# Gates made in two groups, a 128-row recurrence, rest rows in two matmuls, and another order of VectorE's work beside an expert

## The chip, the cores and the metric

The kernel runs on one core of a Trainium2 chip (trn2). The metric is the device time of one execution in microseconds. The engines are TensorE (PE; PEld is its weight load), VectorE (DVE), ScalarE (ACT), GpSimd (POOL) and SyncE (SP), which here only issues DMAs.

## What is computed

An mLSTM recurrence, then a mixture of experts with a capacity, then a dense layer pair with a leaky activation:

```python
# q, k, v, o_gate: (4, 8, 768, 40); i_gate, f_gate: (4, 8, 768)
for t in range(S):
    m_new = max(f[t] + m, i[t]);  fs = exp(f[t] + m - m_new);  ist = exp(i[t] - m_new);  m = m_new
    C = fs * C + ist * outer(v[t], k[t]);  n = fs * n + ist * k[t]
    y[t] = sigmoid(o[t]) * (C @ q[t]) / max(|n . q[t]|, 1)
# x = y as (3072, 320); logits = x @ w_gate (320, 8)
# tokens go to experts greedily by falling logit, 384 tokens an expert
# out[mask] = relu(x[mask] @ w1[e]) @ w2[e]          (320 -> 1024 -> 320)
# then h = x @ w_in; (max(h,0) + alpha*min(h,0)) @ w_out   (320 -> 2048 -> 320)
```

## The kernel before

The sequence is cut into 6 chunks of 128 positions; with 4 batches there are 24 tiles (T = 4c + b) of 128 tokens and 8 heads. The program is written engine by engine, each with its own instruction order, and held together by semaphores. A `Chain` makes an engine wait for its own earlier result.

**Gates.** VectorE scans the gates of all 32 (batch, head) rows over 768 positions (lines 984 to 1012), ScalarE takes two Exps (845, 846), TensorE turns the results (568) and VectorE copies them. GpSimd clears the tiles' buffers and makes constants (420 to 469) before its first product. The decay exponents need the peak in three bf16 parts (`peak3`), one matmul against a selecting column each (588).

**Recurrence.** `over_chunks` runs a step for each tile: chunk 0 written out, chunks 1 to 4 in a loop, chunk 5 written out. In a step TensorE makes the decay exponents and scores of the next tile (`front`, 588 and 595), then for this tile the product with the carried state (617), the state's update (623), the router of two tiles ago (606) and the products with v (633), and turns the previous tile's row (642). ScalarE makes the decays (861), copies turned rows and sends them (868 to 872), and casts a sixteenth of `w_in` and `w_out` to the high part (899 to 903); its queue issues these raw weights, four loads a chunk (`load_raw`). VectorE makes probs (1039), the sum and the state (1059 to 1068) and the row x (1073 to 1079). GpSimd weighs v (478), masks (484), fades the state (490) and makes low parts (498 to 506). SyncE loads a tile with nine DMAs (383 to 387) once it has been used up. Head pairs lie in partitions 0 to 39 and 64 to 103. The o gates come in six large loads on ScalarE's queue and get a Sigmoid each before the rest.

**Routing.** VectorE turns the logits into two integer keys (1100 to 1120). In ten rounds compare (1138, 1140) -> count (667) -> blocks (1146) -> sum (673) -> flag (1155) -> base (679) the limit is found at which an expert is full; then its tokens are listed (1178 to 1217), their rows fetched by indirect DMA (532) and its weights loaded (406 to 410). The rounds of the next expert run between the matmuls of the one that is computed.

**Expert.** Every product of two fp32 matrices is made of fp32r parts, high times high, low times high and high times low: `parts3` (726 to 728) is three matmuls. The feature size 320 is two blocks of 128 and a rest of 64. On the way up the rest block holds high part and low part in its two halves, so it takes two matmuls (742, 743). The first layer's output product `down1` has three output tiles of 128 columns, the third being the rest twice, and each takes `parts3`. An expert has 8 steps of the first layer (`up`, `down1`) and 16 of the second (`up`, `down2`). ScalarE takes Relu and casts to the high part, VectorE makes the low part (`split_hidden`, 1266, 1271, 1276). At the end of an expert VectorE also makes the next keys (`reopen`, `best`), the low parts of the next expert's weights (`low_in` 1246 and 1248, `low_out` 1254) and rows (`rows_lo` 1258). TensorE turns the next expert's rows in three parts through one bank (`turn_rows`, 720), the next part only once `rows_lo` of the one before is done; then comes `first_up`.

```python
if more and 9 <= j < 12:
    low_in(e + 1, j - 9)
if more and 12 <= j < 15:
    rows_lo(e + 1, j - 12)
if more and 12 <= j < 15:
    low_out(e + 1, j - 12)
```

## Time and profile before

| | us |
|---|---|
| three runs | 891.87, 900.04, 902.94 (median 900.04) |
| the profiled execution | 891.99 |
| its span, first to last instruction | 890.1 |
| TensorE busy | 782.2 (88%) |
| VectorE busy | 597.9 (67%) |
| ScalarE busy | 318.0 (36%) |
| GpSimd busy | 166.9 (19%) |
| recurrence, to the last logits | 0 to 196.6 |
| first routing and first fetch | 196.6 to 248.6 |
| each of the six middle experts | 80.2 to 80.3 |

Durations come from the one profiled execution. Matmuls overlap, so the time from one start to the next is what counts, not the duration of one. The idle time that a row shows in square brackets lies before it, and the name behind the arrow is what ended it.

### The profile page before, as it was taken

How to read it: one execution, taken by the hardware profiler on the slowest of the kernel's cores; microseconds unless marked ns; L12 is line 12 of the kernel's file. 1: busy time of each engine (PE TensorE's matmuls, PEld its weight loads, DVE VectorE, ACT ScalarE, POOL GpSimd, SP SyncE). 2: the span in 40 equal slices, each digit the busy share in tenths (PEclk: the TensorE clock that was granted, in tenths of full speed). 3: DMA queues.
4: the chain of work that ended last, by engine and by line, in shares of the span. 5: the costliest groups of instructions: out<-in, count | busy, mean ns of one | idle time of the engine just before them, and what ended most of it. 6: DMA issues, size and time to landing. Idle time of an engine off the chain costs nothing.

```text
span 890.1 us, 16834 instructions
## 1 busy us (share of the span) xinstructions
PE 782.2 (88%) x5518; PEld 725.4 (82%) x5518; DVE 597.9 (67%) x1465; ACT 318.0 (36%) x732; POOL 166.9 (19%) x241
## 2 busy tenths in 40 slices
PE   1979999972199989998998999899989989998995
PEld 1878899961088978897897889889978988897995
DVE  7647678856766785777677677767766786775342
ACT  5426555510122441343235134313522441343331
POOL 8427667600100011011001101100110011011001
PEclk9989999975589999999999999999999999999998
DMA  9788887510500400050041005002300400050000
GB/s 250 157 203 193 205 195 173 136 36 1 168 1 1 143 28 23 7 163 22 0 133 35 22 0 159 24 7 67 101 22 0 141 27 22 1 167 23 1 1 22
DMA packets 102510, 68.52 MB, mean 77 GB/s; under 512 B 67984, under 2 KB 92048, under 8 KB 102480
## 3 DMA queue, kind: packets, MB, share of 16 engines
q1 hardware_dynamic: 85872, 45.05, 20.0%
q10 hardware_dynamic: 13920, 14.42, 5.5%
q0 software_dynamic: 2688, 8.65, 3.1%
q8 instruction: 17, 0.28, 0.1%
q14 instruction: 13, 0.11, 0.0%
HBM read 59.46 MB, written 8.65 MB: 77 GB/s over the span
## 4 chain that ended last, share of the span: by engine, by line
PE 51%; DVE 20%; issue 11%; ACT 8%; SPq 4%; DMA 3%; ACTq 1%; POOL 1%; DVEq 0%; POOLq 0%
PE bank L726 12%; PE bank L728 9%; PE bank L727 9%; DVE g_act L1271 6%; ACT h_hi L952 4%; PE bank L595 4%; PE bank L633 4%; PE bank L742 3%; PE bank L743 2%; DMA s<-w 2%; DVE w_lo L1254 2%; PE bank L667 2%; PE bank L617 2%; DVE by_row L1208 1%; PE bank L606 1%
## 5 line engine op out<-in xcount | busy, mean ns | idle before, releaser
L952 ACT CAST h_hi<-g_act 128x384 fp32r<-128x384 f32 x128 | 65.7, 514 | 188.3 <-DVE g_act L1271 188.3
L726 PE MATMUL bank<-wo_hi,h_hi 128*128 128x320 f32 x384 | 122.8, 320 | 0.6 <-DVE h_lo L1276 0.6
L728 PE MATMUL bank<-wo_hi,h_lo 128*128 128x320 f32 x384 | 120.1, 313 | 0.0
L727 PE MATMUL bank<-wo_lo,h_hi 128*128 128x320 f32 x384 | 119.5, 311 | 0.0
L532 POOL DMA_INDIRECT xe<-x_rows,idx_in x24 | 27.9, 1161 | 451.7 <-DVE idx_in L1216 393.3
L1276 DVE TENSOR_TENSOR h_lo<-g_act,h_hi 128x384 fp32r<-128x384 f32 x128 | 71.5, 559 | 59.8 <-ACT h_hi L952 58.0
L1271 DVE SCALAR_TENSOR_TENSOR g_act<-g_neg,rest_alpha,bank 128x384 f32<-128x384 f32 x128 | 78.3, 612 | 21.8 <-ACT g_neg L950 20.6
L726 PE MATMUL bank<-yT_hi,wi_hi 128*128 128x384 f32 x256 | 92.1, 360 | 0.1
L948 ACT ACTIVATE h_hi<-bank 128x384 fp32r<-128x384 f32 x64 | 31.5, 492 | 169.4 <-PE bank L743 169.4
L728 PE MATMUL bank<-yT_hi,wi_lo 128*128 128x384 f32 x256 | 86.6, 338 | 0.0
L727 PE MATMUL bank<-yT_lo,wi_hi 128*128 128x384 f32 x256 | 86.6, 338 | 0.0
L726 PEld LDWEIGHTS bank<-wo_hi,h_hi 128*128 128x128 f32 x384 | 73.4, 191 | 1.0 <-DVE h_lo L1276 0.9
L727 PEld LDWEIGHTS bank<-wo_lo,h_hi 128*128 128x128 f32 x384 | 73.4, 191 | 0.0
L728 PEld LDWEIGHTS bank<-wo_hi,h_lo 128*128 128x128 f32 x384 | 73.3, 191 | 0.0
L950 ACT ACTIVATE g_neg<-bank 128x384 f32<-128x384 f32 x128 | 62.6, 489 | 29.4 <-PE bank L743 28.7
L726 PE MATMUL bank<-h_hi,w_hi 128*128 128x384 f32 x192 | 69.9, 364 | 0.0
L728 PE MATMUL bank<-h_hi,w_lo 128*128 128x384 f32 x192 | 64.7, 337 | 0.0
L727 PE MATMUL bank<-h_lo,w_hi 128*128 128x384 f32 x192 | 64.4, 335 | 0.0
L543 POOL DMA_INDIRECT out<-out_sb,idx_out x24 | 27.3, 1138 | 190.0 <-DVE out_sb L1334 185.1
L861 ACT ACTIVATE decay<-bank,aT 128x128 f32<-128x128 f32 x192 | 51.5, 367 | 13.8 <-PE bank L588 9.6
L595 PE MATMUL bank<-q_wide,k_in 128*128 128x256 f32 x192 | 52.0, 418 | 1.6 <-DVE probs L1039 1.6
L726 PE MATMUL bank<-xT_hi,w_hi 128*128 128x384 f32 x128 | 51.6, 403 | 1.2 <-DVE xT_lo L1258 1.2
(208 smaller groups left out, 1776.8 us busy)
## 6 DMA issues: line engine op xcount, KB each, us to landing
s<-w SPq DMA_DIRECT2D x8, 1280.0 KB, 9.3
s<-w SPq DMA_DIRECT2D x8, 1024.0 KB, 5.4
s<-w SPq DMA_DIRECT2D x24, 256.0 KB, 6.5
sig<-o ACTq DMA_DIRECT2D x6, 640.0 KB, 8.5
q_in<-qT SPq DMA_DIRECT2D x48, 80.0 KB
q_wide<-qT SPq DMA_DIRECT2D x48, 80.0 KB
k_in<-kT SPq DMA_DIRECT2D x48, 80.0 KB
k_row<-k SPq DMA_DIRECT2D x48, 80.0 KB
```

What stands on the lines that cost most here:

```text
L532: pool.indirect_dma_start(xe[:, t, :], None, x_rows[:, :], bass.IndirectOffsetOnAxis(ap=idx_in[:, t:t + 1], axis=0)).then_inc(rows_in, 16)
L595: ins = pe.matmul(SCORE[y // 2][:, 2 * P * (y % 2):2 * P * (y % 2) + 2 * P], k_in[:, b, y, :], q_wide[:, b, y, :, :].rearrange("p u t -> p ...
L633: ins = pe.matmul(YB[:, D1 * h:D1 * h + D1], probs[:, n, half, y, :], v_in[:, b, h, :], start=True, stop=True)
L726: pe.matmul(acc, ah, bh, start=start, stop=False, skip_group_check=True)
L727: pe.matmul(acc, ah, bl, start=False, stop=False, skip_group_check=True)
L728: return pe.matmul(acc, al, bh, start=False, stop=stop, skip_group_check=True)
L861: ins = act.activation(decay[:, half, y, :], LOGD[half][:, P * y:P * y + P], ACT.Exp, bias=aT[:, c, h:h + 1])
L948: act.activation(h_hi[:, k % 3, :], acc, ACT.Relu).then_inc(act_ready, 1)
L950: act.activation(g_neg[:, k % 3, :], acc, ACT.Relu, scale=-1.0).then_inc(act_ready, 1)
L952: act.copy(h_hi[:, k % 3, :], g_act[:, k % 3, :]).then_inc(g_hi, 1)
L1271: dve.scalar_tensor_tensor(out=g_act[:, n, :], in0=g_neg[:, n, :], scalar=rest_alpha[:, j:j + 1], in1=acc, op0=ALU.mult, op1=ALU.add).then ...
L1276: dve.tensor_tensor(h_lo[:, n, :], g_act[:, n, :], h_hi[:, n, :].bitcast(F32), ALU.subtract).then_inc(h_ready, 1)
```

## The change

- **Gates**: the 32 rows of a chunk lie under each other, 4 chunks in 128 partitions (group 0) and 2 in 64 (group 1). Group 0 is made first; group 1's steps are put between the first four tiles. ScalarE places `peak3`. Tile 0's buffers are cleared by VectorE, the others by GpSimd ahead of its constants.
- **Recurrence**: a head pair lies in partitions 0 to 79, and buffers have 128 rows with zeros below; `own_half` takes each half's own columns of the update. A tile's loads are k_in in one DMA, q_wide in two, k_row in whole runs, v_in, q_in in two (not in chunk 0), and the o gate of the tile. SyncE also issues the raw weights, one or two DMAs a tile. The Sigmoid becomes (1 + tanh(o/2))/2, with a Tanh per tile.
- **Rest rows**: `w2_hi` holds the rest's high part and behind it its low part; `down1` takes two matmuls for the third tile, and both halves of its output are split again for the second layer, with `wi_mix` as the second weight.
- **VectorE's order**: keys of the first 20 tiles are made within chunk 5; beside an expert `reopen` and the first part of `best` come at j = 8, the second at 9, `low_in` at 10 to 12, `low_out` at 13, 14 and after the next expert's first split. ScalarE casts the rows before the last w2 part.

```diff
-    PD = P
+    PD = 2 * D
...
-                for half, at_row in enumerate((0, ODD)):
-                    rows = slice(at_row, at_row + D)
-                    sp.dma_start(q_in[rows, b, :, :], qT[c, b, half]).then_inc(tile_in[b], 16)
-                    sp.dma_start(q_wide[rows, b, :, half, :], qT[c, b, half]).then_inc(tile_in[b], 16)
-                    sp.dma_start(k_in[rows, b, :, :], kT[c, b, half]).then_inc(tile_in[b], 16)
-                    sp.dma_start(k_row[:, b, :, at_row:at_row + D], k[c, b, :, half]).then_inc(tile_in[b], 16)
-                sp.dma_start(v_in[:, b, :, 0:D], v[c, b]).then_inc(tile_in[b], 16)
...
+                sp.dma_start(k_in[0:PD, b, :, :], kT[c, b].rearrange("u d y s -> (u d) y s")).then_inc(qk_in[b], 16)
+                for half in range(2):
+                    sp.dma_start(q_wide[D * half:D * half + D, b, half, :, :], qT[c, b, half]).then_inc(qk_in[b], 16)
+                sp.dma_start(k_row[:, b, 0:DM], k[c, b].rearrange("p u y d -> p (u y d)")).then_inc(kv_in[b], 16)
+                sp.dma_start(v_in[:, b, :, 0:D], v[c, b]).then_inc(kv_in[b], 16)
+                if not first(T, B):
+                    for half in range(2):
+                        sp.dma_start(q_in[D * half:D * half + D, b, :, :].rearrange("d (a u) s -> d a u s", u=2),
+                                     qT[c, b].rearrange("u d (a n) s -> n d a u s", n=2)[half]).then_inc(q_rows_in[b], 16)
+                    sp.wait_ge(x_ready, T - B + 1)
+                sp.dma_start(gate_o[:, b, :], o[T]).then_inc(o_in[b], 16)
...
+            def load_raw(c, b):
+
+                i = B * (c - 1) + b // 2 * 2
+                fs = bass.ds(PW * i, 2 * PW)
+                if b % 2 == 0:
+                    sp.dma_start(wi_raw[:, :, fs], w_in[0:2 * P, fs].rearrange("(t p) f -> p t f", p=P)).then_inc(raw_in[b], 16)
+                    sp.dma_start(wo_raw[:, bass.ds(i, 2), :],
+                                 w_out[bass.ds(P * i, 2 * P), :].rearrange("(j p) d -> p j d", p=P)).then_inc(raw_in[b], 16)
+                else:
+                    sp.dma_start(rest_raw[0:REST, fs], w_in[2 * P:DM, fs]).then_inc(raw_in[b], 16)
+                    sp.dma_start(rest_raw[REST:P, fs], w_in[2 * P:DM, fs]).then_inc(raw_in[b], 16)
+
...
+                if first(T, B) and b == 3:
+                    turn_gates(1)
...
-                        ins = parts3(ACC[t][:, 0:CAP], (w2_hi[:, j, ds], w2_lo[:, j, ds]),
-                                     (h_hi[:, j % 3, :], h_lo[:, j % 3, :]), j == 0, j == J1 - 1)
+                        if t < 2:
+                            ins = parts3(ACC[t][:, 0:CAP], (w2_hi[:, j, ds], w2_lo[:, j, ds]),
+                                         (h_hi[:, j % 3, :], h_lo[:, j % 3, :]), j == 0, j == J1 - 1)
+                        else:
+                            pe.matmul(ACC[t][:, 0:CAP], w2_hi[:, j, ds], h_hi[:, j % 3, :], start=(j == 0), stop=False, skip_group_check=True)
+                            ins = pe.matmul(ACC[t][:, 0:CAP], w2_hi[:, j, ds], h_lo[:, j % 3, :], start=False, stop=(j == J1 - 1),
+                                            skip_group_check=True)
...
+            def gate(c, b):
+                T = B * c + b
+                act.wait_ge(o_in[b], 16 * (c + 1))
+                act.activation(gate_o[:, b, :], gate_o[:, b, :], ACT.Tanh, scale=0.5).then_inc(tanh_ready, 1)
...
+            def gate_sums(g):
+
+                n = HB * len(GROUPS[g])
+                gc.link(dve.tensor_tensor_scan(cum_f[0:n, g, :], ones_row[0:n, :], gate_f[0:n, g, :], 0.0, ALU.mult, ALU.add))
+                gc.link(dve.tensor_tensor(log_in[0:n, g, :], gate_i[0:n, g, :], cum_f[0:n, g, :], ALU.subtract))
+                gc.link(dve.tensor_tensor_scan(peak[0:n, g, :], log_in[0:n, g, :], log_in[0:n, g, :], NEG, ALU.max, ALU.max))
+                for c in GROUPS[g]:
+                    if c == 0:
+                        continue
+                    src, at = bh_rows(c - 1), (c - 1) // 4
+                    gc.link(dve.scalar_tensor_tensor(out=carry[bh_rows(c), g:g + 1], in0=peak[src, at, P - 1:P], scalar=carry[src, at:at + 1],
+                                                     in1=cum_f[src, at, P - 1:P], op0=ALU.max, op1=ALU.add))
+                dve.tensor_scalar(neg_peak[0:n, g, :], peak[0:n, g, :], carry[0:n, g:g + 1], -1.0, ALU.max, ALU.mult).then_inc(gate_logs, 1)
...
+                ch.mark(dve.memset(assigned[:, :, :], 0.0))
+                make_keys(ch, slice(0, NT - B))
+                choose(ch, slice(0, NT - B))
...
             def low_out(e, t):
                 js = slice(3 * t, min(3 * t + 3, J1))
                 dve.wait_ge(whi_ready, 6 * e + t + 4)
-                dve.tensor_tensor(w2_lo[:, js, :], s2[:, js, :], w2_hi[:, js, :].bitcast(F32), ALU.subtract).then_inc(wlo_ready, 1)
+                dve.tensor_tensor(w2_lo[:, js, :], s2[:, js, 0:2 * P], w2_hi[:, js, 0:2 * P].bitcast(F32), ALU.subtract)
+                dve.tensor_tensor(w2_hi[:, js, DM:3 * P], s2[:, js, 2 * P:DM], w2_hi[:, js, 2 * P:DM].bitcast(F32),
+                                  ALU.subtract).then_inc(wlo_ready, 1)
 
...
-                    dve.tensor_tensor(yT_lo[:, t, :], ACC[t][:, 0:CAP], yT_hi[:, t, :].bitcast(F32), ALU.subtract).then_inc(y_ready, 1)
+                    if t < 2:
+                        dve.tensor_tensor(yT_lo[:, t, :], ACC[t][:, 0:CAP], yT_hi[:, t, :].bitcast(F32), ALU.subtract).then_inc(y_ready, 1)
+                    else:
+                        dve.tensor_tensor(yT_lo[REST:P, 2, :], ACC[2][0:REST, 0:CAP], yT_hi[0:REST, 2, :].bitcast(F32),
+                                          ALU.subtract).then_inc(y_ready, 1)
...
+                    if route and j == 8:
+                        reopen(ch)
+                        choose_value(ch, slice(0, NT))
                     if route and j == 9:
-                        reopen(ch)
-                    if route and j == 10:
-                        best(ch)
-                    if more and 9 <= j < 12:
-                        low_in(e + 1, j - 9)
+                        choose_tie(ch, slice(0, NT))
+                    if more and 10 <= j < 13:
+                        low_in(e + 1, j - 10)
                     if more and 12 <= j < 15:
                         rows_lo(e + 1, j - 12)
-                    if more and 12 <= j < 15:
-                        low_out(e + 1, j - 12)
+                    if more and 13 <= j < 15:
+                        low_out(e + 1, j - 13)
                 if more:
                     split_hidden(e + 1, 0)
+                    low_out(e + 1, 2)
```

Three places show how instructions move. First, GpSimd from its first instruction of the kernel on, before:

```order
L420 MEMSET v_in 128x32
L421 MEMSET q_in 128x2048
L422 MEMSET q_wide 128x4096
L423 MEMSET k_in 128x2048
L424 MEMSET k_row 128x1664
L425 MEMSET fade 128x96
L426 MEMSET state 128x1312
L427 MEMSET ident 128x128
```

and after, up to the first clearing for tile 2 (`sel` is the selecting matrix of `peak3`):

```order
L465 MEMSET ident 128x128
L466 ISA
L466 AFFINE_SELECT ident<-ident 128x128
L468 MEMSET sel_114 128x32
L470 AFFINE_SELECT sel_114<-sel_114 128x32 x2
L472 AFFINE_SELECT sel_114<-sel_114 128x32
L474 MEMSET k_in 128x512
L475 MEMSET q_wide 128x1024
L476 MEMSET k_row 128x4x48
L477 MEMSET v_in 128x32
L479 MEMSET k_in 128x512
```

What cleared all four tiles, state included, stands behind the identity and the selector now; tile 0's part is gone from this engine, and the state's clearing comes later.

Second, TensorE in the first layer, one `down1` (bank0 to bank2 are its three output tiles) and what comes next, before:

```order
L726 MATMUL bank0<-h_hi_96,w2_hi_103 128x384
L727 MATMUL bank0<-h_lo_97,w2_hi_103 128x384
L728 MATMUL bank0<-h_hi_96,w2_lo_104 128x384
L726 MATMUL bank1<-h_hi_96,w2_hi_103 128x384
L727 MATMUL bank1<-h_lo_97,w2_hi_103 128x384
L728 MATMUL bank1<-h_hi_96,w2_lo_104 128x384
L726 MATMUL bank2<-h_hi_96,w2_hi_103 128x384
L727 MATMUL bank2<-h_lo_97,w2_hi_103 128x384
L728 MATMUL bank2<-h_hi_96,w2_lo_104 128x384
L667 MATMUL bank6<-choice_51,by_row_88 128x32 x6
L726 MATMUL bank3<-xT_hi_90,w1_hi_101 128x384
```

and after:

```order
L805 MATMUL bank0<-h_hi_96,w2_hi_103 128x384
L806 MATMUL bank0<-h_lo_97,w2_hi_103 128x384
L807 MATMUL bank0<-h_hi_96,w2_lo_104 128x384
L805 MATMUL bank1<-h_hi_96,w2_hi_103 128x384
L806 MATMUL bank1<-h_lo_97,w2_hi_103 128x384
L807 MATMUL bank1<-h_hi_96,w2_lo_104 128x384
L848 MATMUL bank2<-h_hi_96,w2_hi_103 128x384
L849 MATMUL bank2<-h_lo_97,w2_hi_103 128x384
L746 MATMUL bank6<-choice_51,by_row_88 128x32 x6
L805 MATMUL bank5<-xT_hi_90,w1_hi_101 128x384
```

The third matmul into bank2 is gone, and the other eight and the count stand as they did.

Third, VectorE at an expert's end, from the low part of hidden block 14 on (`s_99` and `s_100` are the raw w1 and w2), before:

```order
L1276 TENSOR_TENSOR h_lo<-g_act,h_hi 128x384
L1257 REGISTER_ALU
L1258 TENSOR_TENSOR xT_lo<-bank,xT_hi 128x384
L1253 REGISTER_ALU
L1254 TENSOR_TENSOR w_lo<-s_100,w_hi 128x1152
L1263 REGISTER_ALU
L1271 SCALAR_TENSOR_TENSOR g_act<-g_neg,rest_alpha,bank 128x384
L1275 REGISTER_ALU
L1276 TENSOR_TENSOR h_lo<-g_act,h_hi 128x384
L1257 REGISTER_ALU
L1258 TENSOR_TENSOR xT_lo<-bank,xT_hi 128x384
```

and after:

```order
L1441 TENSOR_TENSOR h_lo<-g_act,h_hi 128x384
L1407 REGISTER_ALU
L1411 TENSOR_TENSOR w_hi<-s_99,w_hi 64x1024
L1422 REGISTER_ALU
L1423 TENSOR_TENSOR xT_lo<-bank,xT_hi 128x384
L1428 REGISTER_ALU
L1436 SCALAR_TENSOR_TENSOR g_act<-g_neg,rest_alpha,bank 128x384
L1440 REGISTER_ALU
L1441 TENSOR_TENSOR h_lo<-g_act,h_hi 128x384
L1422 REGISTER_ALU
L1423 TENSOR_TENSOR xT_lo<-bank,xT_hi 128x384
```

The last `low_in` (`w_hi`) has come in front of the first `xT_lo`, and the `low_out` (`w_lo` from `s_100`, 128x1152) that stood between the first and the second `xT_lo` has gone behind the second.

## Rows read from the trace of the kernel before

**Rows 1.** Windows: busy time of each engine in two stretches, then clock and DMA
```profile
core 0: us, PE busy (x) PEld busy (x) DVE busy (x) ACT busy (x) POOL busy (x), PEclk, DMA share, GB/s
100.00:166.90 66.90, 66.09 (x559) 63.31 (x557) 51.79 (x117) 37.07 (x134) 46.87 (x71) 0.98 0.76 182
331.00:411.30 80.30, 76.82 (x525) 70.91 (x524) 57.13 (x142) 27.39 (x52) 7.30 (x7) 0.98 0.18 53
```

**Rows 2.** Timeline of the first 31 us: start us, duration us, engine, line, operation
```profile
start us, us, engine line op out<-in xcount [idle before <-releaser]
6.49 1.75 DVE L992 TENSOR_TENSOR_SCAN cum_f<-not_first,gate_f 32x768 f32<-32x768 f32 x1 [3.76 <-DMA gate_f<-f_gate]
...
10.56 0.35 SPq L383 DMA_DIRECT2D q_in<-qT  x1
...
18.69 0.91 POOL L468 TENSOR_SCALAR_AFFINE_SELECT own_block<-own_block 128x32 bf16<-128x32 bf16 x1
...
21.83 1.01 PE L588 MATMUL bank<-peak,sel 128*128 128x128 bf16 x8 [0.76 <-issue]
...
22.50 1.28 ACT L861 ACT_TABLE_LOAD   x1 [1.81 <-PE bank L588]
...
30.38 1.92 PE L633 MATMUL bank<-v_in,probs 128*128 128x41 f32 x16
```

**Rows 3.** Timeline of TensorE: the turning of a tile's row, at the end of steps
```profile
48.26 0.52 PE L642 MATMUL bank<-ident,x_sb 128*128 128x128 f32 x3
...
53.69 1.03 PE L588 MATMUL bank<-peak,sel 128*128 x8 [4.91 <-DMA v_in<-v]
...
61.96 0.53 PE L642 MATMUL bank<-ident,x_sb 128*128 128x128 f32 x3
...
106.38 0.53 PE L642 MATMUL bank<-ident,x_sb 128*128 128x128 f32 x3
...
112.97 0.53 PE L642 MATMUL bank<-ident,x_sb 128*128 128x128 f32 x3
...
166.89 0.53 PE L642 MATMUL bank<-ident,x_sb 128*128 128x128 f32 x3
```

**Rows 4.** Timeline of TensorE: the first count of the routing
```profile
202.50 0.34 PE L667 MATMUL bank<-choice,by_row 128*128 128x32 bf16 x6 [5.89 <-DVE by_row L1138]
```

**Rows 5.** Timeline of TensorE at the end of the second expert
```profile
401.37 0.33 PE L743 MATMUL bank<-yT_lo,wi_hi 128*128 128x384 f32 x1
...
405.48 0.55 PE L720 MATMUL bank<-ident,xe 128*128 128x128 f32 x3 [2.46 <-DVE xT_lo L1258]
...
408.88 0.80 PE L720 MATMUL bank<-ident,xe 128*128 128x128 f32 x3 [0.56 <-DVE xT_lo L1258]
...
411.13 0.34 PE L743 MATMUL bank<-xT_lo,w_hi 128*128 128x384 f32 x1
```

**Rows 6.** Waits of VectorE from 53 to 196 us
```profile
engine line waited for: us in total, times, longest us
DVE carried L1059 <- PE bank L633: 20.3, 16, 3.4
```

**Rows 7.** Groups of instructions by line: busy us, mean ns, idle before
```profile
L617 PEld LDWEIGHTS bank<-state,q_in 128*128 128x128 f32 x160 | 21.2, 193 | 2.2 <-DVE hsum L1060 1.0
L623 PEld LDWEIGHTS bank<-vw,k_row 128*104 128x104 f32 x160 | 16.6, 172 | 0.3
...
L1146 DVE TENSOR_TENSOR blocks<-bank,own_block 128x32 fp32r<-128x32 f32 x80 | 15.4, 192 | 37.5 <-PE bank L667 37.5
```

**Rows 8.** Timeline of TensorE: two neighbouring matmuls of the first layer's output product
```profile
355.80 0.33 PE L727 MATMUL bank<-h_lo,w_hi 128*128 128x384 f32 x1
355.97 0.34 PE L728 MATMUL bank<-h_hi,w_lo 128*128 128x384 f32 x1
```

**Rows 9.** Timeline of VectorE at the end of the second expert
```profile
391.04 0.62 DVE L1271 SCALAR_TENSOR_TENSOR g_act<-g_neg,rest_alpha,bank 128x384 f32<-128x384 f32 x1 [0.31 <-ACT g_neg L950]
...
404.87 0.56 DVE L1258 TENSOR_TENSOR xT_lo<-bank,xT_hi 128x384 fp32r<-128x384 f32 x1 [0.55 <-ACT xT_hi L941]
405.34 1.35 DVE L1254 TENSOR_TENSOR w_lo<-s,w_hi 128x1152 fp32r<-128x1152 f32 x1
406.61 0.61 DVE L1271 SCALAR_TENSOR_TENSOR g_act<-g_neg,rest_alpha,bank 128x384 f32<-128x384 f32 x1
...
408.28 0.55 DVE L1258 TENSOR_TENSOR xT_lo<-bank,xT_hi 128x384 fp32r<-128x384 f32 x1
```

525 lines of the change are left out of this document (307 added, 218 removed).

## Prediction

> **What bounds the kernel now.** I read the windows first. In a stretch of the recurrence and in a whole expert the TensorE is busy 95 to 99% of the time, VectorE 71 to 77% [rows 1]; the span is 890.1 us of an execution that took 891.99. So the recurrence and the experts are TensorE's, and only four kinds of gap are not. The order of time shows them. First, TensorE's first useful matmul of the recurrence starts at 21.83 us and tile 0's products with v at 30.38 [rows 2]. Second, the chunk loop has steps that are longer than the rest: between the 16 steps of the loop 118.6 us pass (48.26 to 166.89), while an undisturbed step takes 6.59 (106.38 to 112.97) [rows 3]; 16 of these are 105.4, so 13.2 us are lost, 7.1 of them in the first step (48.26 to 61.96), where TensorE sat 4.91 us until a load had landed. Third, between the last logits and the first count there are 5.89 us in which VectorE makes keys [rows 4]. Fourth, at each expert's end TensorE waits twice for the low half of the next expert's rows [rows 5].
>
> **The start.** Before, VectorE's chain over 32 x 768 gates starts at 6.49 with a scan of 1.75 us, and SyncE may load its first tile only at 10.56, behind GpSimd's memsets [rows 2]. After, the chain works on 128 x 128, the first tile is cleared by VectorE itself, and its loads go out behind four small gate loads. I take one sixth of the first scan's length for what depends on elements, some 0.5 us a scan and 0.2 a small operation, about 2 us in all, from 5.5 us on; two Exps, three transposes and three short copies follow, and the first decay matmul is at about 9 to 10 us. That is not what counts: GpSimd has to finish its constants before its first product and mask. Before, it ends them at 19.6 [rows 2]; after, it has tile 0 less to clear and the padding of k alone, so it ends at about 18, and a weighing and two masks (2 us) later TensorE can run tile 0's last matmuls, at about 19.5 instead of 30.38. I take **-11.0**; the bounds are -7 (GpSimd ends as late as before and the first loads are slow) and -14.
>
> **What the split gates cost.** The second group's sums, splits, diagonals and copies now lie on VectorE inside the first four tiles, some 4.5 us of operations of 0.2 to 0.5 us. VectorE has a little over 1 us free in a step: it waited 20.3 us in 16 steps for y, 3.4 at most [rows 6]. I put 1.5 us of it in TensorE's way, 1.0 for the ten small matmuls of the second group, and 2.0 at tile 4, where the carried product waits for the fades, which VectorE copies only after tile 3's row is made: **+4.5** (bounds +1 and +8).
>
> **The loop's lost time.** Of the first step's 7.1 us I expect 6 back, since the o gates (six large loads ahead of everything) now come tile by tile and the keys' rows in whole runs. The other 6.1 us of the loop lie at the steps where ScalarE issues four raw-weight loads between two tiles' decays; step 10 is the largest (the 9.8 us before 106.38). These issues move to SyncE, past no compute. I take 5 of 6.1. Together **-11.0** (bounds -2 and -13). SyncE now issues seven or eight loads and one or two raw ones a tile, at 0.4 to 0.8 us some 6 us against steps of 6.6, and behind the wait for x; what is queued there is the next tile's load, which has two steps of time. ScalarE gets a tanh for every tile, but loses the four loads; I price it at nothing, hidden beside TensorE's 6.6 us, and at 0.5 us a tile (10 us) if that cover is gone.
>
> **128 rows in the update.** The update's weight load grows from 104 columns (172 ns) to 128 (193 ns as in the carried product) [rows 7]. 8 loads, 20 tiles, 21 ns more are 3.4 us if every load is exposed; some are hidden, **+2.6**.
>
> **The end of the recurrence.** Ten step tables (2.7 us) come after tile 20 and fifteen key operations (about 4.3) after tile 22, where VectorE's waits are the 1.3 us of a mean step and the 3.4 of the longest [rows 6]: **+1.7** (0 to +4). What is left after the last logits are 12 operations on 32 elements at 0.2 us (a 128x32 one took 0.192) [rows 7], 2.5 us and the compare: 3.6 instead of 5.89, **-2.3**. Before the first expert ScalarE's w2 casts shrink by a sixth and 256 KB less are loaded: **-1.5** (0 to -2.5).
>
> **Two matmuls for the rest rows.** In the first layer's product the third output tile takes two matmuls instead of three: 8 x 8 = 64 are gone. Start to start one takes 0.17 us (355.80 to 355.87) [rows 8], its 0.33 being overlapped; 64 x 0.1735 = **-11.1**. VectorE waits there for the counts, 37.5 us in 80 [rows 7], so it isn't what the step waits for. The extra copy for yT_lo lies on ScalarE beside VectorE's subtraction of the same length (bounds -8 and -12).
>
> **The expert's end.** TensorE's last matmuls of two neighbouring up products start at 401.37 and 411.13, 9.76 apart, with waits of 2.46 and 0.56 for xT_lo [rows 5]. VectorE is full from 391.04 on [rows 9]. In the new order the waits in front of 391.04 (0.31) and in front of the first xT_lo (0.55, ScalarE casts w2 before the rows) vanish, since other work is moved into the one and the casts are exchanged: the first xT_lo comes 1.1 us earlier, at 403.75. Between the first and the second xT_lo stood a w2 subtraction (405.34 to 406.61, 1.27 us), which moves behind the second: 408.28 becomes 405.9, 2.4 earlier. TensorE follows that one directly (0.60 later), so the boundary is 2.4 shorter. The w2 work comes back after the third xT_lo and pushes the next compare to within 0.3 us of its count: 2.3 x 7 = **-16.1**. Bounds: 0 (other VectorE work takes the place) and -30 (4.3 a boundary, when both waits and the matmuls at the lower granted clock behind them vanish).
>
> **The sum** is -11.0 + 4.5 - 11.0 + 2.6 + 1.7 - 2.3 - 1.5 - 11.1 - 16.1 = -44.2, against 891.99: 847.8 us. The three runs shown have their median 8 us above that execution and their lowest at its time; I put a quarter of this on top: **850 us**.
>
> **A rule weighed.** The first tile's decays stand behind a table load of 1.28 us [rows 2], the fourth that ScalarE makes by then, since Sigmoid and Exp alternate. Were one needed at each change between Exp and the gate's function, 48 of them would put 61 us on ScalarE; with half of it hidden beside TensorE that is +31 us, 881. The Trainium skill ("ScalarE: Activation LUTs", section "Table sets: the hidden batching unit") says that tables are loaded by set and that Exp and Tanh are in one set, so that the price would be one load in all. No row here shows Tanh; by this rule the sum stays.
>
> **Rivals.**
> (a) The wait at the expert's end only changes its place: VectorE's total work is the same, and it is full for 14 us. For it: nothing but the 0.31 and 0.55 is idle on VectorE, and three w2 pieces still come before the next compare. Against: 1.27 us leave the chain ahead of the second xT_lo. 847.8 + 16.1 + 2 = **866**.
> (b) The start is no earlier than before by more than 3 us, by GpSimd's constants or a first load that lands late: 850 + 8 = **858**.
> (c) Both gaps at the expert's end close fully (-30 instead of -16): **836**.
> (d) Slower than before: loads bound the loop. A tile needs 960 KB, a sixteenth of the raw weights 352 KB and the x rows 192 KB, 1.54 MB per 6.7 us or 229 GB/s, where the stretch from 100 to 167 us moved 182 GB/s at 76% of the engines [rows 1]. At 182 a step is 8.5 us, +28 in 16 steps: 878. If the step also stalls as the first one did (+7.1 each [rows 3]), the whole gain is gone from 6.2 such steps on, and at 8 of 16 the time is 850 + 57 = **907**. Against it: small pieces of k are gone, and each load has two steps of time.
> (e) ScalarE's table loads, above: **881**.
>
> **How the numbers follow.** Forecast 58%; (a) 14%, (b) 11%, (c) 11%, (d) 4% (half of it slower than before), (e) 2%. Around the forecast the bounds of the terms add to about 14 us each way, and the runs spread by some 5. The range 832 to 869 takes in (a), (b) and (c). A difference of 2% or 18 us is about what a measurement of this kernel can tell from no change; only (d) and (e) come near: faster 0.95, same 0.03, slower 0.02.
>
> **What would show it.** Start: first decay matmul at 9 to 11 us and tile 0's products with v at 19 to 21. Loop: 16 steps of about 6.7 with no step over 10 and TensorE without a wait for a load; tile 4 with a wait of some 2 us for the fades. Keys: under 4 us between the last logits and the first count. Experts: 76.6 us each instead of 80.3, of which 1.4 by matmuls and 2.3 by waits; TensorE's waits for xT_lo down from the 3.0 us shown to under 2 an expert. The prediction is wrong if a wait of the loop for loads, or VectorE's compare behind the out copies, is at the top of the waits.

## The result and the profile after

The changed kernel takes 848.5 us, the median of four runs (846.6 to 850.9); the kernel before took 895.9 us beside it (four runs, 891.5 to 902.9). The ratio is 0.9465, with a 95% interval of 0.9386 to 0.9545. Forecast were 850 us, 832 to 869. The profiled execution took 847.56 us with a span of 845.5, so 44.4 us less than the 891.99 of before.

The stages, cut at the same instructions in both profiled executions:

| Stretch | before, us | after, us | change | forecast |
|---|---|---|---|---|
| start to tile 0's products with v | 30.38 | 20.46 | -9.9 | -11.0 |
| from there to the first step of the loop | 17.88 | 19.96 | +2.1 | +2.5, and a part of the update |
| 16 steps of the loop | 118.63 | 109.69 | -8.9 | -6.4 (-11.0, +2.6, +2.0 at tile 4) |
| rest of the recurrence | 26.69 | 27.29 | +0.6 | +1.7 |
| last turned row to first count | 8.92 | 6.94 | -2.0 | -2.3 |
| first count to first expert | 46.15 | 45.21 | -0.9 | -1.5 |
| experts, to the end of the span | 641.45 | 615.95 | -25.5 | -27.2 |

The windows of the changed kernel, one in the loop and one over the second expert, against [rows 1]:

```profile
core 0: us, PE busy (x) PEld busy (x) DVE busy (x) ACT busy (x) POOL busy (x), PEclk, DMA share, GB/s
93.10:150.11 57.01, 57.01 (x486) 55.27 (x485) 41.14 (x99) 36.52 (x128) 42.38 (x61) 1.00 0.82 220
304.50:381.30 76.80, 74.64 (x517) 68.55 (x517) 56.76 (x145) 27.38 (x53) 7.36 (x7) 1.00 0.17 52
```

TensorE has no idle time left in the loop, at 220 GB/s of transfers where before there were 182. The timeline of the start, against [rows 2]:

```profile
2.69 1.28 ACT L927 ACT_TABLE_LOAD   x1 [2.69 <-issue]
...
5.12 0.42 DVE L1089 TENSOR_TENSOR_SCAN peak<-log_in 128x128 f32<-128x128 f32 x1
...
6.31 3.87 DVE L1096 TENSOR_SCALAR neg_peak<-peak,carry 128x128 f32<-128x128 f32 x1
...
6.95 1.80 POOL L481 MEMSET q_in<- 128x2048 f32 x1
8.70 1.19 POOL L482 MEMSET state<- 128x1312 f32 x1
9.83 0.23 POOL L483 MEMSET half_ones<- 128x160 f32 x1
...
15.74 0.74 POOL L535 TENSOR_TENSOR vw<-v_in,wT 128x328 f32<-128x328 f32 x1
17.29 1.23 POOL L541 TENSOR_SCALAR_AFFINE_SELECT probs<-probs 128x512 f32<-128x512 f32 x2 [0.81 <-DVE probs L1191]
...
20.46 1.91 PE L712 MATMUL bank<-v_in,probs 128*128 128x41 f32 x16
```

The scan takes 0.42 us and GpSimd is through with its constants at 15.8, both as fast as forecast or faster. What is late is one row, L1096: 3.87 us for an operation on 128 x 128 elements whose neighbours take 0.2 to 0.4. It ends at 10.18, when GpSimd's row of memsets has ended. So the first decay matmul comes at 11.77 and not at 9 to 11. GpSimd's mask then waits for VectorE, not the other way round.

TensorE in the loop, against [rows 3], and at the first count, against [rows 4]:

```profile
40.42 0.83 PE L721 MATMUL bank<-ident,x_sb 128*128 128x128 f32 x3
...
48.84 0.53 PE L721 MATMUL bank<-ident,x_sb 128*128 128x128 f32 x3
...
55.59 0.53 PE L721 MATMUL bank<-ident,x_sb 128*128 128x128 f32 x3
...
184.34 0.32 PE L746 MATMUL bank<-choice,by_row 128*128 128x32 bf16 x6 [3.91 <-DVE by_row L1301]
```

The step of 13.7 us is one of 8.42 now, and the other 15 are 6.75 each: of 13.2 us of lost time 1.67 is left. That rest is no wait. TensorE was busy throughout the step, and the windows show its clock (here with TensorE's columns alone: us, PE busy, PEclk, DMA share, GB/s):

```profile
40.42:44.70 4.28, 4.28 (x22) 0.60 0.83 208
44.70:48.84 4.14, 4.14 (x39) 1.00 0.95 242
```

A granted clock of 0.60 over 4.28 us costs 1.7 us, the whole excess. In the 20 us before it TensorE had been idle for 0.2 us only, and here it ran at its lower level (1.2 GHz) for most of the stretch. In the kernel before, the first long step holds such a loss too: of its 7.1 us over an undisturbed one 4.91 are the wait for v, and nearly all the rest is the half clock at which the matmuls behind that wait ran (from 53.69 to about 58 us).

The end of the second expert, TensorE first, against [rows 5], then VectorE, against [rows 9]:

```profile
381.27 0.55 PE L799 MATMUL bank<-ident,xe 128*128 128x128 f32 x3 [1.33 <-DVE xT_lo L1423]
383.39 0.55 PE L799 MATMUL bank<-ident,xe 128*128 128x128 f32 x3 [0.26 <-DVE xT_lo L1423]
```

```profile
379.40 1.22 DVE L1411 TENSOR_TENSOR w_hi<-s,w_hi 64x1024 fp32r<-64x1024 f32 x1
380.66 0.56 DVE L1423 TENSOR_TENSOR xT_lo<-bank,xT_hi 128x384 fp32r<-128x384 f32 x1
...
382.79 0.55 DVE L1423 TENSOR_TENSOR xT_lo<-bank,xT_hi 128x384 fp32r<-128x384 f32 x1
```

The waits are 1.33 and 0.26 us instead of 2.46 and 0.56, the second xT_lo follows the first by 2.1 us instead of 3.4, and no w2 piece stands between them. An expert takes 76.7 us instead of 80.3. The boundary of [rows 5] is a disturbed one, though: behind its first wait the clock fell (0.79 on the mean from 404 to 412 us), and the slower matmuls hid a part of the second wait. At the next boundary of before, with the full clock, the two are 2.48 and 1.53 us, 4.01 together and not 3.0:

```profile
489.32 0.55 PE L720 MATMUL bank<-ident,xe 128*128 128x128 f32 x3 [1.53 <-DVE xT_lo L1258]
```

So 2.4 us of waits are gone at a boundary. The clock itself has little part in the shorter expert: before, one takes 80.1 to 80.2 us from a boundary with the full clock on and 80.4 from one without.

### The profile page after: what moved, and what is told of

Read it like the earlier page. It is cut to its first block, busy times and chain, and to the rows that moved or that the text cites. A ratio compares the mean times of both kernels' runs of the same rounds, so it can differ in the third digit from the quotient of the medians.

```text
span 845.5 us, 16938 instructions
## 1 busy us (share of the span) xinstructions
PE 768.7 (91%) x5446; PEld 713.1 (84%) x5446; DVE 586.9 (69%) x1503; ACT 321.6 (38%) x775; POOL 164.2 (19%) x245
## 4 chain that ended last, share of the span: by engine, by line
PE 56%; DVE 25%; issue 10%; ACT 6%; DMA 1%; DVEq 0%; POOL 0%; SPq 0%; ACTq 0%; POOLq 0%
PE bank L805 11%; PE bank L807 9%; PE bank L806 8%; DVE g_act L1436 7%; ACT h_hi L1041 5%; PE bank L665 5%; PE bank L712 5%; PE bank L823 3%; PE bank L824 2%; PE bank L700 2%; PE bank L693 2%; PE bank L746 2%; PE bank L676 2%; DVE by_row L1371 2%; DVE w_lo L1409 1%
## 5 line engine op out<-in xcount | busy, mean ns | idle before, releaser
L589 POOL DMA_INDIRECT xe<-x_rows,idx_in x24 | 23.4, 974 | 445.1 <-DVE idx_in L1379 388.4
L1039 ACT ACTIVATE g_neg<-bank 128x384 f32<-128x384 f32 x128 | 62.4, 488 | 25.5 <-PE bank L824 25.2
L600 POOL DMA_INDIRECT out<-out_sb,idx_out x24 | 30.2, 1259 | 168.6 <-DVE out_sb L1505 163.7
L805 PEld LDWEIGHTS bank<-yT_hi,wi_hi 128*128 128x128 f32 x256 | 48.1, 188 | 4.4 <-DVE yT_lo L1462 2.0
L665 PE MATMUL bank<-q_wide,k_in 128*128 128x256 f32 x192 | 49.6, 404 | 1.0 <-DVE probs L1191 1.0
L712 PE MATMUL bank<-v_in,probs 128*128 128x41 f32 x384 | 48.6, 288 | 0.0
L806 PEld LDWEIGHTS bank<-yT_lo,wi_hi 128*128 128x128 f32 x256 | 48.2, 188 | 0.0
```

The lines of the kernel that those rows point to most:

```text
L600: pool.indirect_dma_start(out[:, :], bass.IndirectOffsetOnAxis(ap=idx_out[:, t:t + 1], axis=0), out_sb[:, t, :], None).then_inc(out_sent, 16)
L665: ins = pe.matmul(SCORE[y // 2][:, 2 * P * (y % 2):2 * P * (y % 2) + 2 * P], k_in[:, b, y, :], q_wide[:, b, :, y, :], start=True, stop=True)
L712: ins = pe.matmul(YB[:, D1 * h:D1 * h + D1], probs[:, n, half, y, :], v_in[:, b, h, :], start=True, stop=True)
L805: pe.matmul(acc, ah, bh, start=start, stop=False, skip_group_check=True)
L806: pe.matmul(acc, ah, bl, start=False, stop=False, skip_group_check=True)
L1039: act.activation(g_neg[:, :], acc, ACT.Relu, scale=-1.0).then_inc(act_ready, 1)
```

## Experiments at the end of an expert

**The old order, put back.** VectorE's and ScalarE's order of before, all else as changed:

```diff
-                    if route and j == 8:
-                        reopen(ch)
-                        choose_value(ch, slice(0, NT))
                     if route and j == 9:
-                        choose_tie(ch, slice(0, NT))
-                    if more and 10 <= j < 13:
-                        low_in(e + 1, j - 10)
+                        reopen(ch)
+                    if route and j == 10:
+                        best(ch)
+                    if more and 9 <= j < 12:
+                        low_in(e + 1, j - 9)
...
-                    if more and 13 <= j < 15:
-                        low_out(e + 1, j - 13)
+                    if more and 12 <= j < 15:
+                        low_out(e + 1, j - 12)
```

> The changed kernel with the expert's end in the order of before, on VectorE (tie choice and reopening after products 9 and 10, the w1 and w2 low parts one product earlier) and on ScalarE (w2 casts ahead of the rows). Theory (the order shortened each boundary): the boundary between two experts' up products goes from 7.1 us back to 9.5, an expert from 76.7 to 79.1, seven of them 17 us, some 865 us. Rival (the wait only moved, and the smaller w2 work alone shortened the boundary): under 5 us, at most 853.

It took 863.3 us (860.1 to 866.0). An expert takes 78.8 us in its trace, 2.1 more than with the new order, and TensorE's wait is back:

```profile
388.12 0.90 PE L799 MATMUL bank<-ident,xe 128*128 128x128 f32 x3 [2.37 <-DVE xT_lo L1423]
```

At the later boundaries, where the clock is full, the second wait is back as well: they are 2.35 and 1.39 us instead of 1.33 and 0.26, so that the two grow by 2.15 us together, which is the 2.1. So the order is worth 7 x 2.1 = 14.7 us; the wait did not only move.

**The third matmul, put back.** Its product is not wanted, so one term of the third output tile is doubled:

```diff
                             pe.matmul(ACC[t][:, 0:CAP], w2_hi[:, j, ds], h_hi[:, j % 3, :], start=(j == 0), stop=False, skip_group_check=True)
+                            pe.matmul(ACC[t][:, 0:CAP], w2_hi[:, j, ds], h_hi[:, j % 3, :], start=False, stop=False, skip_group_check=True)
```

> The changed kernel with a third matmul again on the third output tile of the first layer's product (it adds the high product once more, so this part of the output is doubled in that term). Theory (a matmul costs its pitch): 64 x 0.1735 = 11.1 us more, an expert 78.1 us instead of 76.7, in all some 860. Rival 1 (TensorE is not the bound there, VectorE's counts are): 0 to 3 us. Rival 2 (a matmul costs its whole 0.33 us): 21 us, 870.

It took 857.7 us (855.5 to 861.2), 9.2 more; an expert takes 77.84, 1.14 more. In a step with a count the added matmul costs its pitch:

```profile
317.48 0.33 PE L849 MATMUL bank<-h_hi,w_hi 128*128 128x384 f32 x1
317.66 0.34 PE L850 MATMUL bank<-h_lo,w_hi 128*128 128x384 f32 x1
```

Over the eight products of an expert it comes to 0.14 us each, not 0.17. Where the rest of it is hidden was not looked for.

Order and matmuls are 2.1 + 1.14 of the 3.6 us that an expert became shorter. Of the 0.35 left, 2.5 us in all, most lies in the same two waits: they are 4.01 us before and 3.74 with the old order back, and what neither run put back are w2's smaller cast and subtraction and the rest rows of yT_lo. That these are the cause was not tried by itself.

**Two attempts to close the rest of the gap.** Both are built on the version with the shorter update (below, 841.8 us). In the first, the subtraction for w1's rest rows, the row of 1.22 us ahead of xT_lo, goes to GpSimd:

```diff
+            def low_rest(e):
+                if not first(e, 1):
+                    pool.wait_ge(rows_in, 16 * CT * (e + 1))
+                pool.wait_ge(whi_ready, 6 * e + 3)
+                pool.tensor_tensor(w1_hi[REST:P, 2, :], s1[REST:P, 2, :], w1_hi[REST:P, 2, :].bitcast(F32),
+                                   ALU.subtract).then_inc(w1_rest, 1)
+                pool.wait_ge(w1_rest, e + 1)
...
             with pool.Fori(0, E - 1) as e:
                 fetch_rows(e + 1)
+                low_rest(e + 1)
                 send_out(e)
```

> The version with the update of 80 columns (841.8 us), and the subtraction for the rest rows of w1 (64 x 1024, 1.22 us on VectorE right ahead of the next expert's first xT_lo) on GpSimd. Theory (what VectorE does ahead of xT_lo sets the boundary): TensorE's wait of 1.33 us for the first xT_lo goes to about 0.1 in each of 7 boundaries, an expert 75.5 us instead of 76.7, in all 833 us. Rival 1 (the wait only moves to the second xT_lo or to the next compare): 840 to 842. Rival 2 (GpSimd's work stretches VectorE's): 842 or more.

It took 856.8 us (856.0 to 858.5), 15 more. Of this some 6 are the first expert's (its piece stood ahead of the first gather of rows: TensorE waited 15.8 us for them instead of 8.9), a fault of the experiment and not of the idea. The idea fails in the others, which take 77.9 us instead of 76.7. GpSimd's row at the end of the second expert:

```profile
377.43 2.39 POOL L600 TENSOR_TENSOR w_hi<-s,w_hi 64x1024 fp32r<-64x1024 f32 x1 [2.43 <-DMA xe<-x_rows,idx_in]
```

And VectorE's timeline of the same time:

```profile
374.82 0.56 DVE L1452 TENSOR_TENSOR h_lo<-g_act,h_hi 128x384 fp32r<-128x384 f32 x1 [0.58 <-ACT h_hi L1056]
...
377.62 2.61 DVE L1452 TENSOR_TENSOR h_lo<-g_act,h_hi 128x384 fp32r<-128x384 f32 x1 [0.58 <-ACT h_hi L1056]
```

The same subtraction on VectorE, 0.56 us at 374.82, takes 2.61 when it starts 0.2 us behind GpSimd's, and is done 0.4 us after it.

In the second attempt VectorE keeps the work but does the rows first:

```diff
-                    if more and 10 <= j < 13:
+                    if more and 10 <= j < 12:
                         low_in(e + 1, j - 10)
                     if more and 12 <= j < 15:
                         rows_lo(e + 1, j - 12)
-                    if more and 13 <= j < 15:
-                        low_out(e + 1, j - 13)
+                    if more and j == 13:
+                        low_in(e + 1, 2)
+                    if more and j == 14:
+                        low_out(e + 1, 0)
                 if more:
                     split_hidden(e + 1, 0)
+                    low_out(e + 1, 1)
                     low_out(e + 1, 2)
```

> The version with the update of 80 columns (841.8 us), and on VectorE the next expert's xT_lo ahead of the rest rows of w1 and of w2's low parts: rows 0, then rows 1 and w1's rest rows, then rows 2 and w2's first piece, the two other pieces behind the first hidden product. Theory (what stands ahead of xT_lo in VectorE's order sets the boundary, and the moved work fits behind it): the first xT_lo 1.2 us earlier, the second and third some 0.9, TensorE's waits at a boundary 0.5 us instead of 1.6, seven boundaries some 7 us, in all about 834 to 836. Rival (VectorE is full there, so that the wait only moves to the second xT_lo or to the next compare): 840 to 842.

It took 845.6 us (845.1 to 849.0, six runs), 4 more than without, and an expert 77.5 us. TensorE's waits at the same boundary:

```profile
375.85 0.55 PE L799 MATMUL bank<-ident,xe 128*128 128x128 f32 x3 [0.72 <-DVE xT_lo L1423]
...
377.10 0.44 PE L805 MATMUL bank<-xT_hi,w_hi 128*128 128x384 f32 x1 [0.71 <-DVE w_hi L1411]
...
382.27 0.44 PE L805 MATMUL bank<-h_hi,w_hi 128*128 128x384 f32 x1 [0.78 <-DVE out_sb L1508]
```

Three waits of 0.7 to 0.8 us in the place of 1.33 and 0.26. This is what rival (a) of the prediction describes, wrong for the change and right one step further: VectorE is full there, and w1's rest rows and the copies of the output are late next.

## Experiments on the loop

**Raw weights on ScalarE's queue again.**

```diff
                 for b in range(B):
                     load_tile(c, b)
-                    load_raw(c, b)
...
-                if b % 2 == 0:
-                    act.wait_ge(raw_in[b], 32 * c)
-                    act.wait_ge(raw_in[b + 1], 32 * c)
+                if b == 0:
+                    act.wait_ge(raw_in[0], 64 * c)
+                    if not isinstance(c, int):
+                        load_raw(c + 1)
```

> The changed kernel with the raw weights of the last layer loaded as before: by ScalarE, four loads per chunk, issued between two tiles' work. Theory (these issues held ScalarE and so the decays): steps longer than 6.75 us come back at the second tile of chunks 1 to 3 and late in chunk 0, 5 us in all, some 853 to 854 us. Rival (the loop's lost time came from small or late loads): all steps stay at 6.75 us, 848.5.

It took 859.1 us (855.7 to 860.2). Three steps, one for each of the chunks named, take 10.27, 10.01 and 10.32 us instead of 6.75. ScalarE's queue in front of one of them, in its timeline:

```profile
51.67 0.42 ACTq L989 DMA_DIRECT2D wi_raw<-w_in  x1
...
53.69 0.97 ACTq L992 DMA_DIRECT2D wo_raw<-w_out  x1
54.79 0.46 ACT L1003 CAST wo_hi<-wo_raw  x1 [2.89 <-issue]
```

ScalarE issues for 3 us, its casts and then the next tile's decays stand behind that, and TensorE behind the decays. Ten us lie in these steps, twice what I expected. Windows of TensorE show why, over the first of them and over two such steps of the kernel before:

```profile
56.42:66.69 10.27, 8.87 (x60) 0.83 0.96 240
```

```profile
68.55:76.53 7.98, 7.04 (x59) 1.00 0.96 215
96.55:106.38 9.83, 8.79 (x60) 0.83 0.98 226
```

The three steps have 1.0 to 1.4 us of idle time each, and behind it the clock falls, to a mean of 0.83: 0.17 x 10.2 = 1.7 us a step, 5.2 of the 10.4. In the kernel before, the same issues made two steps at full clock, 1.4 and 1.2 us too long, and one with the lower clock, 3.2 too long. The issues themselves thus cost under 2 us a step, and the clock 1.7 more where it falls. It does not fall each time: with both changes of the next runs at once there is such a step of 8.43 us at full clock. The first long step, 13.7 us before, does not come back: the step there is 8.98, without idle time and at a clock of 0.75.

**The keys in short runs.** One transfer of whole rows becomes two of runs of 160 bytes, as before:

```diff
-                sp.dma_start(k_row[:, b, 0:DM], k[c, b].rearrange("p u y d -> p (u y d)")).then_inc(kv_in[b], 16)
+                for n in range(2):
+                    sp.dma_start(k_row[:, b, 0:DM].rearrange("p (a n d) -> p n a d", n=2, d=D)[:, n, :, :],
+                                 k[c, b].rearrange("p u y d -> p (u y) d").rearrange("p (a n) d -> p n a d", n=2)[:, n, :, :]).then_inc(kv_in[b], 16)
```

> The changed kernel with the keys' rows loaded in two transfers of runs of 160 bytes per tile, as before, instead of one of whole rows (the same bytes and places). Theory (short runs and raw loads on ScalarE's queue made the 13.7 us step together): little alone, all steps but the one after tile 4 stay at 6.75 us, 848 to 850 us. Rival (the short runs alone filled the queues): a wait for v of several us in the first steps, over 852 us.

It took 861.0 us (860.3 to 864.2): the rival's total, though not in the place where either put it. The long steps are not near tile 4 but later: 11.86, 8.42, 10.04 and 10.12 us. SyncE's queue tells why. One tile's issues in the changed kernel's timeline:

```profile
64.27 0.35 SPq L396 DMA_DIRECT2D k_in<-kT  x1
...
65.59 0.36 SPq L399 DMA_DIRECT2D k_row<-k  x1
...
70.65 0.35 SPq L396 DMA_DIRECT2D k_in<-kT  x1
```

And in this kernel's, from one tile's first issue to that of the seventh after it:

```profile
71.41 0.33 SPq L396 DMA_DIRECT2D k_in<-kT  x1
...
72.96 1.34 SPq L400 DMA_DIRECT2D k_row<-k  x2
...
128.87 0.35 SPq L396 DMA_DIRECT2D k_in<-kT  x1
```

The keys' issues take 1.34 us of the queue instead of 0.36. From 71.41 to 128.87 lie seven tiles of issues, 8.2 us each, against steps of 6.75: SyncE falls behind by 1.5 us a tile, until its lead is used up and TensorE waits for q_wide, 5.6 us in three waits. The rest of the 13.4 us by which the four long steps exceed 6.75 is lower clock (0.71 on the mean in the longest step, 0.80 to 0.83 in the others), behind the three waits and, in the step of 8.42, without a wait of its own. In the changed kernel the issues of the tile shown take 6.4 us of 6.75, and those of a tile with the other kind of raw loads 6.5 to 6.9. That queue is as good as full, which no row of busy time tells, since issuing isn't counted as busy.

**Both at once.** 

> Both at once: raw weights on ScalarE's queue and keys in short runs. Theory (together they made the 13.7 us step of before): the steps around tile 3 and 4 show TensorE waiting for v, some 5 us more than with the raw loads alone (859.1), about 864 us. Rival (it was the six loads of the o gates, 3.9 MB ahead of everything, or the later start): no more than with the raw loads alone.

It took 856.3 us (853.1 to 857.5), no more than either alone. With the raw loads gone from SyncE its queue has room for the short runs. No step takes over 10.1 us, so the 13.7 of before needs something else. The theory that the two together made it is out.

**SyncE's queue as before.** The kernel just named, and:

```diff
+            sp.wait_ge(consts, 4)
             for b in range(B):
                 load_tile(0, b)
...
-                if not first(T, B):
+                if True:
                     for half in range(2):
                         sp.dma_start(q_in[D * half:D * half + D, ...
```

> The kernel of the last run (raw weights on ScalarE's queue, keys in short runs), with SyncE's queue as before in two more things: its first load waits for GpSimd's constants (some 10.6 us), and the carried product's q rows are loaded in the first chunk too, so that tile 5's loads are issued late, behind the raw weights' 1.4 MB. Theory: this makes the 13.7 us step of before: TensorE waits over 3 us for v or q near tile 4 or 5 and one step there takes over 11 us. Rival (it was the six loads of the o gates ahead of everything): no step near tile 4 over 10.3 us. The start is some 5 us later either way.

It took 868.2 us (two runs). The step is there, 12.44 us long, with a wait of 4.04 us in it, where before had 13.7 and 4.91 [rows 3]:

```profile
48.41 0.53 PE L724 MATMUL bank<-ident,x_sb 128*128 128x128 f32 x3
53.43 3.42 PE L668 MATMUL bank<-q_wide,k_in 128*128 128x256 f32 x8 [4.04 <-DMA q_wide<-qT]
60.85 0.53 PE L724 MATMUL bank<-ident,x_sb 128*128 128x128 f32 x3
```

The last of the raw loads' issues and the q loads behind it:

```profile
44.61 0.60 ACTq L996 DMA_DIRECT2D wo_raw<-w_out  x1
...
45.32 0.87 SPq L398 DMA_DIRECT2D q_wide<-qT  x2
```

The q loads that TensorE waits for go out at 45.32, right behind 1.4 MB of raw weights, and it resumes at 53.43. The other 1.7 us of the step are lower clock (0.86 on the mean). The long step thus came of a queue that started late and had eight q loads more in the first chunk, so that a tile's loads ran into the burst; neither the burst alone nor the short runs with it made it. Which of the two it takes, the late start or the q loads, was not separated, nor whether it takes the short runs.

**The o gates of all tiles first**, into a place that nobody reads, their data not used:

```diff
+            o_rows = o.rearrange("c p n -> p c n")
+            for c in range(NCH):
+                to = wo_raw[:, B * c:B * c + B, :] if c < 4 else wi_raw[:, c - 4, 0:B * DM].rearrange("p (b n) -> p b n", b=B)
+                act.dma_start(to, o_rows[:, B * c:B * c + B, :]).then_inc(o_early, 16)
```

> The changed kernel with six more loads ahead of everything on ScalarE's queue: the o gates of all tiles (3.9 MB), into tiles that are not used until chunk 1, as before; their data is not used. Theory of the prediction (these loads made the long first step): a wait for a load of several us in tiles 1 to 5 and a step over 10 us. Rival (they only delay the start): the first products with v 3 to 10 us later than 20.46, and steps as in the changed kernel.

It took 860.5 us (two runs). The first decay matmul starts at 24.89 us instead of 11.77, the products with v at 33.57, and of the loop's steps the first takes 7.88 us, with a wait of 0.89 for the fades, and the other 15 take 6.75. No wait is for a load. The rival holds: by themselves these loads only delay the start, here by 13.1 us, more than the rival gave them, since the input gates stand behind them on the same queue.

**The update with the 80 columns it uses.**

```diff
-                    pe.matmul(UPD[:, 2 * D1 * y:2 * D1 * (y + 1)], k_row[:, b, 2 * D * (y // 2 + 2 * (y % 2)):2 * D * (y // 2 + 2 * (y % 2)) + P],
+                    pe.matmul(UPD[0:PD, 2 * D1 * y:2 * D1 * (y + 1)], k_row[:, b, 2 * D * (y // 2 + 2 * (y % 2)):2 * D * (y // 2 + 2 * (y % 2)) + PD],
```

> The changed kernel with the state update's weights cut from 128 to the 80 columns that are used. Theory (a weight load costs time by its columns and is exposed in the update): 48 columns fewer are some 20 ns more than the 24 from 104 to 128 (21 ns) gave, so 42 ns less for each of 8 x 20 loads, up to 6.7 us; steps of 6.4 instead of 6.75, 842 us. Rival (the steps are 6.75 for another reason, the loads are hidden behind the matmuls): 0 to 1 us.

It took 841.8 us (839.1 to 842.4), ratio to the kernel before 0.9356 (0.9271 to 0.9442). It is the fastest of all, 6.7 us below the changed kernel. A step is 6.43 us instead of 6.75, and the groups by line from 50 to 165 us show it (count, busy us and mean ns). The changed kernel's:

```profile
L700 PEld LDWEIGHTS bank<-vw,k_row 128*128 128x128 f32 x120 | 14.6, 192 | 0.0
```

This kernel's:

```profile
L700 PEld LDWEIGHTS bank<-vw,k_row 128*80 128x80 f32 x120 | 9.8, 149 | 0.0
```

0.32 us over 8 loads are 40 ns for 48 columns, all of it exposed. The Trainium skill ("TensorE: Matmul & The Clock Gate", section "LDWEIGHTS (loading the stationary operand)") gives a load's time as its columns over 1.2 in ns, whatever the rows. By this section of the Trainium skill 48 columns are an estimated 40 ns, which the step's 40 and the rows' 43 bear out.

## Experiments on the start

**The long row by two tensors.**

```diff
-                dve.tensor_scalar(neg_peak[0:n, g, :], peak[0:n, g, :], carry[0:n, g:g + 1], -1.0, ALU.max, ALU.mult)
+                dve.scalar_tensor_tensor(out=neg_peak[0:n, g, :], in0=peak[0:n, g, :], scalar=carry[0:n, g:g + 1],
+                                         in1=minus_one[0:n, :].to_broadcast([n, P]), op0=ALU.max, op1=ALU.mult)
```

> The changed kernel with the row -max(peak, carry) (3.87 us beside GpSimd's memsets) made by an operation with two tensor operands (a column of -1 repeated) instead of one. Theory (a one-tensor operation on VectorE waits until GpSimd's memsets leave it a gap, two-tensor ones do not): 0.3 us instead of 3.87, the first decay matmul at 8.3 us instead of 11.8; tile 0's products with v gain less, since GpSimd's constants then end last (15.8 us, then 0.7 and 0.6 us): 2 to 2.5 us earlier. Rival 1 (the operation waited for data or for something else in front of it): it stays near 3.9 us. Rival 2 (GpSimd's memsets stretch anything on VectorE): near 3.9 us too, but the scans of 0.42 us beside the same memsets speak against it.

The timeline of its start:

```profile
6.24 0.35 DVE L1098 SCALAR_TENSOR_TENSOR neg_peak<-peak,carry,minus_one 128x128 f32<-128x128 f32 x1
6.62 0.45 DVE L1106 CAST peak_parts<-neg_peak 128x128 bf16<-128x128 f32 x1
...
6.93 1.88 POOL L482 MEMSET q_in<- 128x2048 f32 x1
7.10 0.29 DVE L1108 TENSOR_TENSOR neg_a<-neg_peak,peak_parts 128x128 f32<-128x128 f32 x1
...
7.43 1.46 DVE L1109 CAST peak_parts<-neg_a 128x128 bf16<-128x128 f32 x1
```

The row falls from 3.87 to 0.35 us, beside the same memsets; the cast behind it, which has one tensor operand, now takes the blow with 1.46 us, until the memset of q_in is over. The two-tensor subtraction between them, inside that memset, takes 0.29. The run with the o gates first shows the old one-tensor row without a neighbour: there the gates come so late that GpSimd is idle, and it takes 0.29 us. Tile 0's products with v start at 17.67, 2.8 us earlier. That fits what the Trainium skill says ("SBUF — State Buffer", section "Who interferes with whom"): VectorE and GpSimd hold one pair of ports exclusively for a whole instruction; copies, casts and operations with scalars can need it, and an operation with two tensors in SBUF collides only with a GpSimd instruction that reads SBUF. The subtraction of 2.61 us beside GpSimd's (above) is the second kind. The Trainium skill speaks of one instruction that blocks; the row of 3.87 us went on through three more memsets, and there the measurement decides.

The time, however, is 848.5 us (848.1 to 849.3), the same as without. The last row of the recurrence is turned at 178.91 us against 177.40: the gain of 2.8 us and 1.5 more are gone by then. Windows of TensorE in this kernel (its clock is the third number from the right):

```profile
36.00:44.00 8.00, 8.00 (x39) 0.57 0.83 233
108.00:112.00 4.00, 4.00 (x23) 0.57 0.89 262
```

The lower clock costs 0.43 x 8 = 3.4 us in the first window and 1.7 in the other, against 1.7 in the one stretch of the changed kernel, which is most of the 4.3 us. Such stretches fall differently in each trace: of the fourteen kept, eleven have one between 36 and 52 us while TensorE is busy, and the other three have none of that kind. Whether an earlier start brings them on or they came by chance is open; no run settles it.

**The best start and the shorter update together**, with GpSimd's constants for the routing moved between the first tiles:

```diff
-            for b in range(B):
-                weigh_values(0, b)
+            weigh_values(0, 0)
+            pool.memset(q_in[:, :, :, :], 0.0).then_inc(wide_zero, 1)
+            weigh_values(0, 1)
+            route_constants()
+            weigh_values(0, 2)
+            block_constants()
+            weigh_values(0, 3)
```

> A version meant to beat both: the changed kernel with the update's weights of 80 columns, the two-tensor operation for the negated row, and GpSimd's routing constants and its clearing of q_in moved between the first four tiles' work. Theory: -6.7 us by the update (841.8 measured), and a start limited no longer by GpSimd's constants: tile 0's products with v 3.5 us earlier than 20.46, in all some 838 us. Rival (the moved constants delay the tiles' masks or the q rows' loads): 842 us or more.

It took 843.5 us (839.2 to 843.7), no faster than the shorter update alone (841.8); the rival's side of the line. Products with v start at 18.13. The cast behind the two-tensor row takes 1.84 us, and the moved constants collide in turn: a 128x8 operation of 0.17 us takes 1.06 beside the moved GpSimd work. Here the clock is full from 20 to 152 us, and the wait for the fades, which the prediction had put at tile 4, does appear, with 0.90 us.

## Why the prediction was right, point by point

- **Start, -11.0 (measured -9.9).** Right in size, by a wrong step, so in part by luck. "GpSimd has to finish its constants before its first product and mask" put the end at 18 us; they end at 15.8, and VectorE's row of 3.87 us set the start instead. "0.2 a small operation" failed for one operation with a busy neighbour.
- **Split gates, +4.5 (measured +2.1 ahead of the loop, against 2.5 forecast).** Of the 2.1 some 0.5 are the update's, so the 1.5 and 1.0 us were too high together; nothing separates them. "2.0 at tile 4, where the carried product waits for the fades" is not in the changed kernel's trace: TensorE has no wait from 40 to 49 us, and the 1.67 us there are lower clock. The wait exists all the same. The run with the third matmul has the same recurrence, and in its trace the clock falls one step later:

```profile
43.12 1.09 PE L693 MATMUL bank<-state,q_in 128*128 128x82 f32 x8 [0.90 <-DVE fade L1127]
```

  That step takes 7.88 us, 1.1 too long, at full clock. Two more runs show the same wait, with 0.89 and 0.90 us. In the changed kernel the slower matmuls ahead of this product cover the wait. The mechanism was right, its price of 2.0 about twice too high, and that 1.67 us stand in its place is luck.
- **The loop's lost time, -11.0 (measured -11.5, the 1.67 us that are left taken off).** The amounts fit the kernel before: of the first step's 7.1 us 5.4 are gone against 6 forecast, and of the other 6.1 all, against 5. The causes were named in part wrongly. For the first step I gave "the o gates (six large loads ahead of everything)" and "the keys' rows in whole runs". The o gates alone make no long step, and the short runs alone make none there; it took SyncE's late queue with more in it and the raw loads' burst. For the steps with raw loads ScalarE's issues are the cause, but the prediction has no term for the clock in the loop, which was 1.7 us of their 6.1 and some 2 of the first step's 7.1, and which makes the 5 us into 10 when the loads are put back.
- **Update, +2.6 for 20 tiles (measured 0.16 us a step, so 3.2 in 20).** The mechanism held, and its reverse, 80 columns, gave 6.7 us. "Some are hidden" did not: 0.16 us over 8 loads are 20 ns each, the whole difference of the rows.
- **Rival (d), loads bound the loop.** It did not come, but one more issue a tile and shorter runs bring it: 8.2 us a tile, as SyncE's time for issuing and not as GB/s; its price took the 182 GB/s of before, and the changed kernel moved 220 in the loop. The prediction's "some 6 us against steps of 6.6" was the right row to watch, and a little low.
- **End of the recurrence, keys and the part before the first expert** (+1.7, -2.3, -1.5; measured +0.6, -2.0, -0.9) were all right within 1.1 us.
- **64 matmuls, -11.1 (measured -9.2)** and **expert end, -16.1 (measured -14.7):** both shown by putting them back; 2.5 us more come from what was not separated. The working took its 3.0 us of waits from the disturbed boundary; its 2.4 came from VectorE's rows and met the 2.4 that the undisturbed ones lost. (The working's "355.80 to 355.87" has a slip: the row is 355.97 [rows 8], which gives the 0.17 that was used.) Rival (c), both gaps closed, was not reached, and the two attempts show why: VectorE is full.
- **The table loads.** One load of 1.28 us is in the trace, and none at a change between Exp and Tanh; rival (e) is out, and the rule of the Trainium skill ("ScalarE: Activation LUTs", section "Table sets: the hidden batching unit") that the two share a set agrees with this trace.
